# Attention and two expert layers on one core: another order of loads, weight products and first operands in the front

## The reference

```python
# attention: q, k, v (2, 8, 768, 64), centroids (8, 16, 64)
q_assign = argmax(normalise(q) @ normalise(centroids).T)      # k_assign likewise
scores = where(q_assign == k_assign, q @ k.T / sqrt(64), -1e9)
x = softmax(scores) @ v                                       # to (1536, 512)
# first layer: w1, w2 (512, 1024), w3 (1024, 1024), w_out (1024, 512)
x = (((x @ w1) * (x @ w2)) @ w3) @ w_out
# second layer: w_in (512, 2048), w_out (2048, 512), alpha (2048)
h = x @ w_in
out = (max(h, 0) + alpha * min(h, 0)) @ w_out
```

## Time and profile before

| | |
|---|---|
| median of 3 runs | 801.8 us (800.17 to 802.02) |
| profiled execution, its own time | 800.21 us |
| its span (first to last instruction) | 798.4 us |
| TensorE busy | 764.2 us (96%) |
| VectorE busy | 429.7 us (54%) |
| ScalarE busy | 334.9 us (42%) |
| GpSimd busy | 188.6 us (24%) |
| moved by transfers | 54.07 MB |

### The profile page before, as it was taken

The page is one execution under the profiler, slowest core; times in us unless marked ns, Lnnn a source line. Parts: engine busy times, 40 slices in busy tenths (PEclk is TensorE's granted clock), DMA queues, the critical chain, the costliest instruction groups (busy, mean ns, idle before and its releaser), DMA issues.

```text
span 798.4 us, 12360 instructions
## 1 busy us (share of the span) xinstructions
PE 764.2 (96%) x4290; PEld 714.2 (89%) x4290; DVE 429.7 (54%) x704; ACT 334.9 (42%) x679; POOL 188.6 (24%) x210
## 2 busy tenths in 40 slices
PE   5999999899899988989999999999999999999998
PEld 4888898798898987889999999999999999999997
DVE  5224988898788887552212115367434444434442
ACT  5124987788788787442212114343121111112111
POOL 2120576867757765410000000000000000000000
PEclk9999999999999999999999999999999999999999
DMA  9734464645645322330000003232000001001001
GB/s 282 161 100 101 109 145 110 134 115 126 133 109 132 90 66 53 100 105 1 1 1 1 0 0 93 90 109 80 1 19 22 1 0 40 0 0 39 1 1 39
DMA packets 63572, 54.07 MB, mean 68 GB/s; under 512 B 31264, under 2 KB 51760, under 8 KB 63536
## 3 DMA queue, kind: packets, MB, share of 16 engines
q1 hardware_dynamic: 63536, 53.59, 26.1%
HBM read 31.50 MB, written 3.19 MB: 43 GB/s over the span
## 4 chain that ended last, share of the span: by engine, by line
PE 70%; POOL 15%; issue 6%; DMA 2%; ACT 2%; DVE 2%; SPq 1%; POOLq 1%; ACTq 0%; DVEq 0%
PE slot L572 55%; PE acc L572 12%; POOL xf L519 3%; POOL xf L515 3%; PE slot L635 2%; POOL xl L525 2%; POOL v L468 1%; DMA xo<-xf 1%; POOL oh L494 1%; POOL v L464 1%; DMA early<-in_moe_w_out 1%; DVE w L1183 1%; POOL c L486 1%; PE slot L686 1%; POOL c L487 1%
## 5 line engine op out<-in xcount | busy, mean ns | idle before, releaser
L572 PE MATMUL slot<-xh,w 128*128 128x384 f32 (+1 forms) x1024 | 276.9, 336 | 0.0
L572 PEld LDWEIGHTS slot<-xh,w 128*128 128x128 f32 x1024 | 186.9, 188 | 2.4
L572 PE MATMUL slot<-xl,w 128*128 (+1 forms) x512 | 172.3, 336 | 0.0
L1020 ACT CAST gh<-gf 128x384 fp32r<-128x384 f32 x64 | 32.9, 514 | 204.2 <-PE acc L572 178.2
L1126 DVE TENSOR_TENSOR pl<-slot,ph 128x384 fp32r<-128x384 f32 x192 | 97.5, 549 | 13.9 <-ACT ph L895 12.6
L1120 DVE TENSOR_REDUCE nm<-slot 128x1 f32<-128x768 f32 x96 | 91.3, 951 | 22.3 <-PE slot L572 21.7
L572 PEld LDWEIGHTS slot<-xl,w 128*128 128x128 f32 x512 | 96.0, 188 | 2.3
L635 PE MATMUL slot<-ident,pf 128*128 128x128 f32 x576 | 82.5, 277 | 14.0 <-DVE pl L1126 13.8
L895 ACT CAST ph<-slot 128x384 fp32r<-128x384 f32 x192 | 83.4, 485 | 28.0 <-PE slot L635 27.1
L887 ACT ACTIVATE pf<-slot,nm 128x768 f32<-128x768 f32 x96 | 87.8, 915 | 15.3 <-DVE nm L1120 15.2
L635 PEld LDWEIGHTS slot<-ident,pf 128*128 128x128 f32 x576 | 67.6, 141 | 24.8 <-DVE pl L1126 19.1
(11 more groups left out here) (121 smaller groups left out, 1115.3 us busy)
## 6 DMA issues: line engine op xcount, KB each, us to landing
stage<-in_moe_w SPq DMA_DIRECT2D x16, 256.0 KB, 3.3
stage<-in_moe_w_in SPq DMA_DIRECT2D x16, 256.0 KB, 2.7
stage<-in_moe_w_out SPq DMA_DIRECT2D x16, 256.0 KB, 3.0
qk<-in_q SPq DMA_DIRECT2D x16, 192.0 KB, 3.7
qk<-in_k SPq DMA_DIRECT2D x16, 192.0 KB, 4.2
vn<-in_v SPq DMA_DIRECT2D x16, 192.0 KB, 3.3
stage<-in_moe_w SPq DMA_DIRECT2D x6, 512.0 KB, 5.3
q<-k SPq DMA_DIRECT2D x16, 192.0 KB, 2.7
```

Source lines behind the costliest of these rows:

```text
L572: return nc.tensor.matmul(o, a, b, start=start, stop=stop)
L1020: copy(gh[j % 2][:, :], gf[j % 2][:, :]).then_inc(gh_done, 1)
```

## The change

All of it is in the front and in the first step.

- SP loads w3 tile 0 and the first quarter of wo behind the centroids, then alpha, the second quarter, w3 tile 1, the other two quarters, w3 tiles 2 and 3, and only then q and k of heads 0 and 1. v of heads 0 and 1 comes behind w3 tiles 4 and 5. The loads of tiles 6 and 7 stand between the copies of the first heads, tile 6 ahead of `stack_second`, tile 7 ahead of the masks.
- TensorE turns w3 tile 0 first; centroids and alpha go to `acc`. Product 0 runs alone: chunks 0 and 1 by parts (`product_first`), each pair of matmuls as soon as its parts are there, then chunks 2 and 3; w3 tile 1 is turned behind them, then come chunks 4 to 7, and product 1 in two halves.
- Operands of head 0 are turned in the middle of product 1, those of head 1 before product 2, the cluster scores run before product 3, the operands of head 2 before product 5. Each tile is turned ahead of the product of the tile before it. ScalarE and VectorE follow with their parts; the loops are written out.
- Even tiles are turned into slot 1, odd ones into slot 2. Score tile 0 waits for the remainder of tile 6, score tile 1 for that of tile 7.

```diff
...
             sp.dma_start(cn[:, :], cen.rearrange("h c d -> (h c) d")).then_inc(ld_cen, 16)
-            load_qk(0, 0)
-            load_v(0, 0)
-            load_v(0, 1)
-            load_qk(0, 1)
-            sp.dma_start(al16[:, :], alpha.rearrange("(j p) -> j p", p=P)).then_inc(ld_al, 16)
             load_w3(0, 0)
+            load_wo(0)
+            sp.dma_start(al16[:, :], alpha.rearrange("(j p) -> j p", p=P)).then_inc(ld_al, 16)
+            load_wo(1)
             load_w3(1, 1)
-            for i in range(NWO):
+            for i in range(2, NWO):
                 load_wo(i)
...
                 sp.dma_start(early[NWO + f - 2][:, :], w3d[f]).then_inc(ld_early[NWO + f - 2], 16)
-            for j in range(2):
-                stack_first(0, j)
-                next_qk(0, j + 2)
+            load_qk(0, 0)
+            load_qk(0, 1)
             for parity in range(2):
...
                 load_w3(4 + parity, parity)
+            load_v(0, 0)
+            load_v(0, 1)
+            for j in range(2):
+                stack_first(0, j)
+                next_qk(0, j + 2)
+            sp.wait_ge(w3_turned, 5)
+            load_w3(6, 0)
             for j in range(2):
                 stack_second(0, j)
+            sp.wait_ge(w3_turned, 6)
+            load_w3(7, 1)
             for j in range(2):
                 masks(0, j)
-            for parity in range(2):
-                sp.wait_ge(w3_turned, 4 + parity + 1)
-                load_w3(6 + parity, parity)
             for f in range(2):
...
                     pe.wait_ge(exp_done, tile(it, c - 1))
+                elif c == 1:
+                    pe.wait_ge(w3_lo, NF)
                 if t == 0:
...
             def turn_w3(f, parity):
-                s = 2 - parity
-                if isinstance(f, int) and f < 4:
-                    source = stage[parity] if f < 2 else early[NWO + parity]
-                    if f < 2:
-                        pe.wait_ge(ld_stage[parity], 16)
-                    else:
-                        pe.wait_ge(ld_early[NWO + parity], 16)
+                s = 1 + parity
+                if f in (2, 3):
+                    source = early[NWO + parity]
+                    pe.wait_ge(ld_early[NWO + parity], 16)
                 else:
                     source = stage[parity]
-                    pe.wait_ge(ld_stage[parity], 8 * (f - parity))
-                if not isinstance(f, int) or f >= 2:
+                    pe.wait_ge(ld_stage[parity], 16 * (f // 2 + 1) if f < 2 else 16 * (f // 2))
+                if f >= 2:
                     pe.wait_ge(w3_lo, f - 1)
...
 
+            def product_first():
+
+                o = slot[0][:, 0, :]
+                pe.wait_ge(piece_hi, 1)
+                pe.wait_ge(w3_hi, 1)
+                for g in range(2):
+                    mm(o, w3h[:, 0, g, :], woh[:, g, :], g == 0, False)
+                pe.wait_ge(piece_lo, 1)
+                for g in range(2):
+                    mm(o, w3h[:, 0, g, :], wol[:, g, :], False, False)
+                pe.wait_ge(w3_lo, 1)
+                for g in range(2):
+                    mm(o, w3l[:, 0, g, :], woh[:, g, :], False, False)
+
             def product_tile(f, parity):
...
             pe.wait_ge(setup_pool, IDENT)
-            for j in range(2):
-                for half in range(2):
-                    turned(0, j, half, True)
+            turn_w3(0, 0)
             pe.wait_ge(setup_act, 1)
-            nc.tensor.transpose(slot[0][0:D, 0, 0:P], cn[:, :], ident[:, :])
+            nc.tensor.transpose(acc[0:D, 0, 0:P], cn[:, :], ident[:, :])
             pe.wait_ge(ld_al, 16)
-            nc.tensor.transpose(slot[0][:, 1, 0:NJ], al16[:, :], ident[0:NJ, 0:NJ]).then_inc(cen_turned, 1)
-            turn_w3(0, 0)
+            nc.tensor.transpose(acc[:, 1, 0:NJ], al16[:, :], ident[0:NJ, 0:NJ]).then_inc(cen_turned, 1)
+            product_first()
+            pe.wait_ge(piece_lo, 2)
+            product_wc(0, (2, 3))
             turn_w3(1, 1)
-            pe.wait_ge(table_done, 2)
-            for i in range(NWO):
+            for i in range(2, NWO):
                 pe.wait_ge(piece_lo, i + 1)
-                for f in range(2):
-                    if i == 0:
-                        pe.wait_ge(w3_lo, f + 1)
-                    product_wc(f, (2 * i, 2 * i + 1))
+                product_wc(0, (2 * i, 2 * i + 1))
             turn_w3(2, 0)
-            turn_w3(3, 1)
-            for half in range(2):
-                cluster(0, 0, half, True)
-            with pe.Fori(2, NF // 2) as i:
-                product_tile(2 * i - 2, 0)
-                turn_w3(2 * i, 0)
-                product_tile(2 * i - 1, 1)
-                turn_w3(2 * i + 1, 1)
+            pe.wait_ge(w3_lo, 2)
+            product_wc(1, range(NF // 2))
+            pe.wait_ge(table_done, 2)
             for half in range(2):
-                turned(0, 2, half, True)
-            pe.wait_ge(w3_lo, NF)
+                turned(0, 0, half, True)
+            product_wc(1, range(NF // 2, NF))
+            for f in range(2, NF - 2):
+                turn_w3(f + 1, (f + 1) % 2)
+                for half in range(2):
+                    if f == 2:
+                        turned(0, 1, half, True)
+                    elif f == 3:
+                        cluster(0, 0, half, True)
+                    elif f == 5:
+                        turned(0, 2, half, True)
+                product_tile(f, f % 2)
+            turn_w3(NF - 1, 1)
+            pe.wait_ge(w3_lo, NF - 1)
             for c in range(LEAD):
...
                 act.wait_ge(w3_turned, f + 1)
-                if not isinstance(f, int) or f >= 2:
+                if f >= 2:
                     act.wait_ge(wc_full, f - 1)
-                copy(w3h[:, parity, :, :], slot[2 - parity][:, :, :].rearrange("p a (g f) -> p (a g) f", g=4)
+                copy(w3h[:, parity, :, :], slot[1 + parity][:, :, :].rearrange("p a (g f) -> p (a g) f", g=4)
                      ).then_inc(w3_hi, 1)
...
             act.wait_ge(setup_pool, OPERANDS)
-            for j in range(2):
-                for half in range(2):
-                    operands_hi(0, j, half, True)
-            w3_hi_part(0, 0)
             wo_hi(0)
+            w3_hi_part(0, 0)
+            wo_hi(1)
+            wo_hi(2)
             w3_hi_part(1, 1)
-            for i in range(1, NWO):
-                wo_hi(i)
-            for f in range(2):
-                w3_hi_part(2 + f, f)
-                wc_copy(f, f)
-            with act.Fori(2, NF // 2) as i:
-                wc_copy(2 * i - 2, 0)
-                w3_hi_part(2 * i, 0)
-                wc_copy(2 * i - 1, 1)
-                w3_hi_part(2 * i + 1, 1)
+            wo_hi(3)
+            w3_hi_part(2, 0)
+            wc_copy(0, 0)
+            for half in range(2):
+                operands_hi(0, 0, half, True)
+            w3_hi_part(3, 1)
             for half in range(2):
-                operands_hi(0, 2, half, True)
+                operands_hi(0, 1, half, True)
+            wc_copy(1, 1)
+            for f in range(2, NF - 2):
+                w3_hi_part(f + 2, f % 2)
+                if f == 4:
+                    for half in range(2):
+                        operands_hi(0, 2, half, True)
+                wc_copy(f, f % 2)
             for c in range(LEAD):
...
                 dve.wait_ge(cen_turned, 1)
-                turned_c = slot[0][0:D, 0, 0:P].rearrange("p (h c) -> p h c", h=H)
+                turned_c = acc[0:D, 0, 0:P].rearrange("p (h c) -> p h c", h=H)
                 ordered(nc.vector.memset(f32(ctab[:, :, :, :]), 0.0))
...
                     ordered(copy(ctab[rows, :, 0, cols], turned_c))
-                copy(al[:, :], slot[0][:, 1, 0:NJ])
+                copy(al[:, :], acc[:, 1, 0:NJ])
                 for rows, cols in halves:
...
                 dve.wait_ge(w3_hi, f + 1)
-                tt_(w3l[:, parity, :, :], slot[2 - parity][:, :, :].rearrange("p a (g f) -> p (a g) f", g=4),
+                tt_(w3l[:, parity, :, :], slot[1 + parity][:, :, :].rearrange("p a (g f) -> p (a g) f", g=4),
                     f32(w3h[:, parity, :, :]), ALU.subtract).then_inc(w3_lo, 1)
...
             dve.wait_ge(setup_pool, OPERANDS)
-            for half in range(2):
-                operands_lo(0, 0, half, True)
-            centroid_table()
-            for half in range(2):
-                operands_lo(0, 1, half, True)
-            w3_lo_part(0, 0)
             wo_lo(0)
-            w3_lo_part(1, 1)
+            w3_lo_part(0, 0)
             wo_lo(1)
-            for i in range(2, NWO):
-                wo_lo(i)
-            w3_lo_part(2, 0)
-            w3_lo_part(3, 1)
+            wo_lo(2)
+            w3_lo_part(1, 1)
+            wo_lo(3)
+            centroid_table()
+            for f in range(2):
+                w3_lo_part(2 + f, f)
+                for half in range(2):
+                    operands_lo(0, f, half, True)
+            w3_lo_part(4, 0)
             for half in range(2):
```

(90 more changed lines are left out.)

6 lines of the change are left out of this document (removed).

## The result

| | before | changed |
|---|---|---|
| median | 801.07 us (798.71 to 803.08, 7 runs) | 795.52 us (794.07 to 796.67, 7 runs) |
| profiled execution, its own time | 800.21 us | 795.52 us |
| its span | 798.4 us | 793.7 us |

The ratio is 0.9929, with a 95% interval of 0.9909 to 0.995: faster, by 0.5 to 0.9%, or 4.0 to 7.3 us. The forecast was 798.5 us, 3.3 us less than the median then known, with a range down to 795.9. In two later comparisons the same changed kernel had ratios of 0.9922 (0.9902 to 0.9942) and 0.9915 (0.9893 to 0.9937). The forecast's own ratio, 798.5 / 801.8 = 0.9959, lies outside all three intervals; the end of its range, 795.9 / 801.8 = 0.9926, lies inside all three. So that the size was missed is no accident; that the time fell just outside the range, and not just inside, may be one.

What follows compares the result with a forecast made beforehand. The prediction took TensorE's delayed front to bound the kernel: score tile 0 at 57.55 instead of 60.89 us gains 3.3 us, so span 798.4 becomes profiled 796.9, plus 1.6 to the median gives 798.5 us. Range 795.9 to 801.5.

Steps and rivals of the forecast that it cites:

- Where the front is slow, and what starts it: Front before score tile 0: whatever starts that tile before 60.89 us moves everything behind it by the same amount.
- Loads: SP's queue at the start: wo's first quarter lands at about 7.0 us, bounds 5.9 and 8.9.
- The 0.65 MB of lag: Load queue: a load lands only when some 0.65 MB queued behind it has moved too.
- The vector chain, six matmuls and one turn: Product 0: 4.68 us from landing to chunks 2 and 3, then matmuls 2.5 and tile 1's turn 1.5, ending at 15.7.
- The new wait: Before chunks 6 and 7: TensorE idles 1 to 2 us for wo 3's remainder; they start at 19.25 us.
- The third rival: Front: waits within product 0 keep the clock at 1.2 GHz up to 19.25 us and beyond; gain 1.3, 800.5 us; chance 0.13.
- What TensorE has left: From chunks 6 and 7 to score tile 0: 38.3 us of work, so that tile can start at 57.55 us.
- The last wait: Before score tile 0: swapped slots turn the 1.71 us wait for w3 tile 7's remainder into nothing.
- Sum: Score tile 0 at 57.55 instead of 60.89 us: 3.3 us gained, 1.7 from the removed wait, 1.6 from earlier product work.
- From the profiled execution to the median: Whole run: 796.9 us for a profiled execution, median 1.6 above it, so 798.5 us.
- The late loads: Start of the front: queued weight loads bring wo's first quarter at 13.6 us, 3.3 us slower, 805; chance 0.10.
- The larger gain: Front: quarter of wo at its lower bound and clock high early; gain 4.8 to 6.2 us, about 796.3; chance 0.16.

Runs made afterwards that it cites:

- the swap alone: Kernel before with only the w3 slots swapped and the wait for tile 7's remainder moved to score tile 1: 801.19 us, ratio 1.0011.
- the kernels with the parts of wo 3 first: Changed kernel, wo 3's parts made ahead of w3 tile 1's on ScalarE and VectorE: 792.29, 792.40 us; with 17 unread transposes before the first product too: 791.96, 791.29 us.
- the filled one: Changed kernel with eight matmuls that nothing reads put in TensorE's idle stretch before chunks 6 and 7: 795.61 us, ratio 0.993.

## Why the prediction was off

*Where the front is slow, and what starts it.* Right. What is gained at the first score tiles reaches the end of the span, apart from the low stretches.

*Loads.* Predicted landing 7.0 us; it came before 6.10 in the changed kernel's first profile, at 6.6 in its second. The landing in the transfer view is 4.4 us after an issue at 1.63, so 6.0: near the lower bound. The 0.65 MB of lag was read from a queue half full of small pieces; a landing at 6.0 leaves, by the same sum, (6.0 - 2.6) us x 386 GB/s = 1.31 MB, a lag of 0.26. That the small pieces made the difference is not shown. ScalarE, which GpSimd's setup held until 6.10, started 0.4 to 0.9 us early.

*The vector chain, six matmuls and one turn.* Chain from ScalarE's start: 10.90 - 6.10 = 4.80 against 4.68. Six matmuls took 2.0 us and the turn 1.04, against 2.5 and 1.5, in the first profile, since the clock rose at about 12 us; in the second profile it rose later and the turn began at 14.1. So chunks 6 and 7 started at 17.45, 18.65 and 17.77 in three profiles against 19.25 predicted.

*The new wait.* Its place, its releaser and its size (2.08 us, predicted 1 to 2) were right. Its consequence was not priced in the sum: the clock fell behind it in two of three profiles, for 1.64 us. The third rival had the clock stay low from the start; instead it rose and fell again.

*What TensorE has left.* Right in sum: 38.3 predicted, 38.08 in the profile without the low stretch. In part that is luck: a group of six operand transposes costs 0.57 us there (24.34 - 23.77), not 0.75, so the term of 2.25 was 0.5 too large, and the other terms were a little too small.

*The last wait.* This step failed in its reasoning. It gave 1.71 us to the slot swap; the swap alone brings nothing (ratio 1.0011), because head 2's operands, still behind tile 7, stop TensorE for 2.14 us. In the whole change these are made before product 5, so the term is 2.1 us, or 2.4 counted from the turn of tile 7. The cover that the prediction named for score tile 1 was the right one, but the wait next in line stood on another semaphore. Missing: 0.4 to 0.7 us.

*Sum.* Score tile 0 was predicted 3.3 us earlier; it came 3.72, 4.16 and 3.40 us earlier, and with the 0.4 us behind it 4.12, 4.57 and 3.80 at tile 1.

*From the profiled execution to the median.* This step, with the range built on it, put the measured time outside. The sum was made against one profiled execution, 800.21 us, and its distance to the median of three runs, 1.6 us, was added to the changed kernel's time as if it belonged to the kernel. Of the 3.0 us between 798.5 and 795.52, this is 1.6: the changed kernel's profiled execution is its median, and in the two repeats it lies within 0.1 us of it. With seven runs the profile of the kernel before lies 0.9 under its median, and a second one, at 805.89 us, 5 us above the median of its twelve. The other 1.4 us lie between the two profiled executions, whose spans are 4.7 us apart and not 3.3: 0.4 at score tile 0, 0.4 behind it (the last wait), 0.6 in the rest, where both have two low stretches.

The range had no term for the clock outside the front. In the second profile of the kernel before, the wait that the change removes cost 1.6 us more, and its front was 1.3 us later. Held against both profiles of before (66.06 and 68.97), the three of the changed kernel (61.94, 61.49, 62.26) give 3.8 to 7.5 us; measured gains were 5.6, 6.0 and 6.8 us.

The executions without a profile have only a mean granted clock. In the profiles 0.998 stands for one low stretch, 0.995 and 0.996 for two, 0.994 for three. At 0.998, the highest seen, the five runs of the kernel before have a median of 798.41 us and the seven of the changed one 793.99, 4.4 us apart. At 0.996 it is 799.96 (16 runs) against 794.22 (4), 5.7 apart, and at 0.994 801.03 (29) against 796.10 (7), 4.9 apart. These groups mix comparisons, and five of the seven runs at 0.998 come from one. So with as many low stretches the change gives 4.4 to 5.7 us, near its front gains of 3.8 to 4.6. Seven of the 19 runs of the changed kernel are at 0.998, and five of the 74 of the kernel before that have a clock on record. One stretch that the change can take away is shown, behind the last wait; that such stretches make up the whole of the other 1 to 2 us is not shown, since no profile was taken of most executions.

*The rivals.* The late loads did not come (the quarter landed at 6.0 to 6.6). The masks were issued at 51.33, as worked out (51.4), and nothing waited for them. The larger gain, given 0.16 and 796.3 us, was nearest.

## What to carry to other kernels

A wait has two prices: its length, and what TensorE's clock does behind it; the second varies between executions, so a sum from one profile should carry it as a term on both sides, for waits that are removed and for waits that are made. For the same reason the distance of one profiled execution from the median is no constant to add: count the low stretches in each profile before two are compared. Before a wait is booked as gone, every semaphore that the next instructions wait on must be followed to what stands in the same engine's list: here the producer of the next operand stood right behind the one that was freed. If a reorder opens a wait elsewhere, it may be as cheap to close: swapping two entries on two engines was worth another 2 to 4 us.

## What the runs showed of the hardware

- The clock fell to the 1.2 GHz level behind waits of TensorE of 1.56 us and more in some executions and not in others of the same kernel: behind the 2.1 us wait of the changed kernel in two of three profiles, behind the 1.71 us wait of the kernel before in one of two. With no wait above 0.5 us from 11 us on (the kernels with the parts of wo 3 first, and the filled one) it did not fall from 14 to 24 us in any of five profiles.
- The length of a wait does not say whether it falls. A wait of 2.36 us had no fall (the changed kernel with the old slots), one of 2.14 had (only the slots). Of the fourteen waits of 1.56 to 1.59 us near 215 us ten had one; the fourteen of 1.72 to 1.75 us near 330 us had none.
- The span behind the front is longer the more low stretches it has: 730.7 and 731.3 us with one, 731.8 to 732.3 with two, 733.3 to 735.1 with three.
- Transposes alone raised the clock: after twelve of them from 1.53 us on, the turn of w3 tile 0 took 1.09 and 1.40 us in two profiles instead of 1.94.
- The granted clock of the view reads 1.00 in 0 to 14 us, where spacings of 0.42 us show the low level; only falls later than that show in it.
